# Attention scores in PSUM: two halves of 288 columns, or 512 and 64 side by side

## What is computed

```python
scores = scale * np.matmul(q, k.transpose(0, 1, 3, 2))
thresh = np.max(scores, axis=-1, keepdims=True) - tau
scores = np.where(scores >= thresh, scores, -1000000000.0)
attn = np.exp(scores - np.max(scores, axis=-1, keepdims=True))
attn = attn / (np.sum(attn, axis=-1, keepdims=True) + 1e-09)
x = np.matmul(attn, v)                  # heads side by side: 2304 x 512

h = x @ w_in                            # 512 -> 2048
x = (h * np.tanh(softplus(h))) @ w_out  # -> 512

g, val = x @ w_gate, x @ w_val          # 512 -> 1536
out = (silu(g) * val) @ w_out2          # -> 512
```

## Time and profile before

| | before |
|---|---|
| median of 3 runs | 1256.94 us (1254.13 to 1261.06) |
| the profiled execution | 1252.67 us |
| its span, first to last instruction | 1250.8 us |
| mean granted TensorE clock | 0.977 |
| TensorE matmul, busy | 1172.3 us, 94% |
| TensorE weight load, busy | 1139.1 us, 91% |
| DVE, ACT, POOL busy | 573.6, 476.1, 530.4 us |

### The profile page before, as it was taken

One profiled execution on the slowest core, in us unless ns is written; L12 is line 12 of the kernel. 1 busy time (PEld: TensorE's weight loads), 2 busy tenths in 40 slices (PEclk: granted clock), 3 DMA queues, 4 the chain that ended last, 5 costly groups with the idle time before them and its releaser, 6 DMA issues.

```text
span 1250.8 us, 21818 instructions
## 1 busy us (share of the span) xinstructions
PE 1172.3 (94%) x8608; PEld 1139.1 (91%) x8608; DVE 573.6 (46%) x1208; ACT 476.1 (38%) x873; POOL 530.4 (42%) x698
## 2 busy tenths in 40 slices
PE   1767689999999999999999998999999999999998
PEld 0656579999999999999999998999999999999998
DVE  3777741566677650355666653035666410002220
ACT  1555454334444244434454324433444304302210
POOL 4455568656677734323434523432443304301210
PEclk9777799999999999999999999999999999999999
DMA  7111147666656555444444454544433455444443
GB/s 240 44 30 44 49 125 250 220 200 204 193 198 186 204 170 168 154 132 144 148 137 141 136 161 137 175 151 143 137 116 120 135 195 178 169 164 162 166 166 106
DMA packets 83253, 190.69 MB, mean 152 GB/s; under 512 B 29392, under 2 KB 29392, under 8 KB 83152
## 3 DMA queue, kind: packets, MB, share of 16 engines
q1 hardware_dynamic: 83152, 189.30, 46.9%
HBM read 148.90 MB, written 40.37 MB: 151 GB/s over the span
## 4 chain that ended last, share of the span: by engine, by line
PE 88%; DVE 4%; ACT 2%; POOL 2%; issue 1%; DMA 1%; SPq 1%; DVEq 0%; ACTq 0%
PE ps_m L451 23%; PE ps_m L453 23%; PE ps_m L452 23%; PE ps_x L508 5%; PE ps_x L522 4%; PE ps_s L477 3%; PE ps_x L523 3%; PE ps_s L478 3%; DVE p_t L711 1%; DVE p_lo_b L723 1%; DMA k_raw<-kt 1%; PE ps_x L504 1%; DVE nmax L703 1%; ACT p_t L625 1%; DVE p_lo L723 1%
## 5 line engine op out<-in xcount | busy, mean ns | idle before, releaser
L451 PE MATMUL ps_m<-x_hi,w_sp 128*128 128x288 f32 x1280 | 379.9, 297 | 6.0 <-ACT g_raw L646 3.4
L453 PE MATMUL ps_m<-x_hi,w_sp 128*128 128x288 f32 x1280 | 378.0, 295 | 0.0
L452 PE MATMUL ps_m<-x_lo,w_sp 128*128 128x288 f32 x1280 | 377.3, 295 | 0.0
L451 PE MATMUL ps_m<-g_hi,w_sp 128*128 128x288 f32 x896 | 265.3, 296 | 0.0
L453 PE MATMUL ps_m<-g_hi,w_sp 128*128 128x288 f32 x896 | 264.2, 295 | 0.0
L452 PE MATMUL ps_m<-g_lo,w_sp 128*128 128x288 f32 x896 | 263.9, 295 | 0.0
L451 PEld LDWEIGHTS ps_m<-x_hi,w_sp 128*128 128x128 f32 x1280 | 240.5, 188 | 8.0 <-ACT g_raw L646 4.3
L453 PEld LDWEIGHTS ps_m<-x_hi,w_sp 128*128 128x128 f32 x1280 | 240.5, 188 | 0.0
L452 PEld LDWEIGHTS ps_m<-x_lo,w_sp 128*128 128x128 f32 x1280 | 240.5, 188 | 0.0
L451 PEld LDWEIGHTS ps_m<-g_hi,w_sp 128*128 128x128 f32 x896 | 168.2, 188 | 0.3
L452 PEld LDWEIGHTS ps_m<-g_lo,w_sp 128*128 128x128 f32 x896 | 168.1, 188 | 0.0
(11 more groups left out here) (79 smaller groups left out, 1548.3 us busy)
## 6 DMA issues: line engine op xcount, KB each, us to landing
w_sp<-scratch SPq DMA_DIRECT2D x204, 512.0 KB, 3.3
scratch<-w_sp SPq DMA_DIRECT2D x68, 512.0 KB, 2.9
w_raw<-weights SPq DMA_DIRECT2D x68, 256.0 KB, 3.4
q_raw<-qt SPq DMA_DIRECT2D x64, 144.0 KB, 3.7
k_raw<-kt SPq DMA_DIRECT2D x64, 144.0 KB, 3.7
out_t<-o_sb SPq DMA_DIRECT2D x16, 288.0 KB, 4.2
v_raw<-v SPq DMA_DIRECT2D x32, 128.0 KB, 2.4
v_raw<-v SPq DMA_DIRECT2D x32, 32.0 KB, 2.8
```

The costliest lines, as they stand in the source:

```text
L451: nc.tensor.matmul(ps, w_h, x_h, start=first, stop=False)
L452: nc.tensor.matmul(ps, w_h, x_l, start=False, stop=False)
L453: return nc.tensor.matmul(ps, w_l, x_h, start=False, stop=last)
```

## The change

The two score places are now seen as one run of 576 columns across two neighbouring banks: 512 columns fill the first bank and 64 lie at the start of the second. The matmuls of a chunk write columns 0 to 511 and 512 to 575 in place of 0 to 287 and 288 to 575 of each bank pair. Their number is the same, four for each head of a chunk, and so is the order of steps on every engine, since the planner's numbers are as before. `rowmax`, `exp` and `mask` take the 576 columns as one contiguous run.

```diff
-        def halves(ap):
-            return ap.rearrange("p (h t) -> p h t", h=2)
-
+        s_flat = ps_s.rearrange("p b t -> p (b t)")[:, 0:SEQ]
+        s_alone = ps_m.rearrange("p b t -> p (b t)")[:, BANK:BANK + SEQ]
...
         def s_banks(C):
             alone = C < CHUNKS * PAIRS
-            return ps_m[:, 1:3, 0:HALF] if alone and C % 2 else ps_s[:, :, 0:HALF]
+            return s_alone if alone and C % 2 else s_flat
...
-                for half in range(2):
-                    to = s_banks(C)[:, half, :]
-                    cols = slice(half * HALF, (half + 1) * HALF)
+                for cols in (slice(0, BANK), slice(BANK, SEQ)):
+                    to = s_banks(C)[:, cols]
                     for e in heads:
                         q = q_sp[:, e, q_columns(e, ci)]
                         nc.tensor.matmul(to, q, k_hi[:, e, cols], start=e == heads[0], stop=False)
...
-                act.activation(halves(p_t[:, slot, :]), s_banks(C), ACT.Exp, bias=nmax[:, slot:slot + 1]).then_inc(e_ready, 1)
+                act.activation(p_t[:, slot, :], s_banks(C), ACT.Exp, bias=nmax[:, slot:slot + 1]).then_inc(e_ready, 1)
...
-                dve.tensor_reduce(nmax[:, slot:slot + 1], s_banks(C), axis=AX.XY, op=ALU.max, negate=True).then_inc(max_ready, 1)
+                dve.tensor_reduce(nmax[:, slot:slot + 1], s_banks(C), axis=AX.X, op=ALU.max, negate=True).then_inc(max_ready, 1)
...
-                p = halves(p_t[:, slot, :])
+                p = p_t[:, slot, :]
```

## The result

The changed kernel takes 1277.28 us in the median of its first four runs, the kernel before 1256.51: a ratio of 1.0163 with a 95% interval of 1.013 to 1.0196. Slower, by 20.8 us. Five more runs of the same kernel gave 1276.91 us and 1.0158 (1.0135 to 1.0181). Every ratio in this document is against executions of the kernel before made beside the run in question, whose medians lay between 1256.4 and 1258.7 us.

What follows compares the result with a forecast made beforehand. PE was taken to bound the middle stage, a chain through all engines the first. 17.8 + 2.8 = 20.6 us on the 1256.94 us median gave 1277.5 us, range 1264 to 1291.

Steps and rivals of the forecast that it cites:

- head-chunk: 128 queries of one head against 576 keys, four score matmuls on PE; forecast 646 to 716 ns at full clock against 530.
- the short slot: PE's start-to-start time after a 64-column score matmul: 110 to 132 ns, because it must hold the next weights' load.
- 188 - 78 = 110 ns: Lower bound for a 64-column matmul's slot: score-weight load duration of 188 ns less 78 ns overlap, taken from the short transposes.
- Middle stage: Later batches' attention woven into the MLP matmuls, 168.2 to 980 us: 118 x 151 ns = 17.8 us longer (13.7 to 21.9).
- the 6.3 us that the prediction read: All the time PE waited while attention was woven into the MLP, none for the score chain; too little to hide the growth.
- First stage: Batch 0's attention alone, 26.8 to 168.2 us, bound by a chain through all engines: 2.8 us longer, bounds 0 to 14.9.
- three head-chunks of ten: Those the chain of waits passes in one pair of heads in batch 0's attention: 0.71 us a pair, times four.
- 0.28 for a half-clock chunk: Growth in us in batch 0's attention where another engine waits: 354 ns less 74 ns of last-matmul latency, 280 ns.
- Contiguous operands: Row maximum, exp and mask reading one run of 576 columns: no gain taken, at most 66 ns per exp, 2.4 us.
- The 60 ns slot: Rival: 64-column score matmuls nearly as cheap as short transposes, 1259 to 1262 us; chance 0.10 together with PE time swallowed by waits.
- columns alone: Rival: PE slots cost only their columns, nothing for the load; 480 ns per head-chunk, up to 9.1 us faster, 1248 us; chance 0.03.
- PE's time disappears in waits: Rival: idle PE time absorbs the longer score matmuls, so no change; chance 0.10 together with the 60 ns case.

Runs made afterwards that it cites:

- the additional matmuls: The kernel before with two unused 64-column matmuls more per head-chunk: 1286.11 us (1.0249) with weights of 128 columns, 1277.23 us (1.0171) with weights of 64.
- the cuts at 384 and 448: The changed kernel's contiguous place, cut as 384 + 192 and as 448 + 128 columns: 1262.06 us (1.0037) and 1268.58 us (1.0095) against the kernel before.
- the alternating order: The changed kernel with its matmuls ordered k_hi 512, k_hi 64, k_lo 512, k_lo 64, so no two short ones follow each other: 1277.50 us, ratio 1.0166.
- the kernel with the new scores in all the rest: 512 + 64 columns for all chunks but the 36 of batch 0, which keep two halves of 288: ratio 1.0125 against the kernel before, +15.7 us.
- Timed alone: 512 + 64 columns for the 36 chunks of batch 0 only, two halves of 288 elsewhere: ratio 1.0048 against the kernel before, +6.0 us.
- 320 + 256: The changed kernel's contiguous place, cut after 320 columns instead of 512: 1255.33 us, ratio 0.999 against the kernel before.
- 64 + 512: The changed kernel with the short matmuls first, columns 0 to 63 ending the first bank and 512 in the second: 1283.58 us, ratio 1.0219.

## Why the prediction was right, and where it was not

The forecast of 1277.5 us met 1277.28, with +20.6 forecast and +20.8 measured. The mechanism was right; that the two agree within 0.2 us is luck, since the difference is known to some 4 us either way (1.013 to 1.0196) and two deviations in a head-chunk cancel.

- **A head-chunk costs 646 to 716 ns, middle 681, +151.** Right: +148 ns in the distance above. The parts: 230 ns for 512 columns (forecast 213 to 226, a little under), 110 ns for 64 (forecast 110 to 132, at its lower end). The two deviations, +2 x 11 against the middle of one and -2 x 11 against that of the other, cancel. The 12 ns over the columns are not a fixed price: slots at full clock were 132 for 288 columns, 175 for 384 and 230 for 512, that is 12, 15 and 17 ns over 0.417 ns a column.
- **What holds the short slot is the load of the next weights.** Right, and shown by the additional matmuls (110 and 57 ns for loads of 128 and 64 columns behind the same 64 moving ones), the cuts at 384 and 448, and the alternating order. The conclusion from 188 - 78 = 110 ns hit the value itself. The sentence that no row shows the load's throughput holds for the rows chosen, not for the trace, as the pair of loads at 276.75 us shows.
- **Middle stage 17.8 us, nothing hides it.** 118 x 148 ns = 17.5 us by the measured growth; 15.7 (12.3 to 19.0) timed, 17.7 (16.2 to 19.2) at equal clock. In the traces it grew by 15.6, 19.3 and 19.7 us (the change twice, then the kernel with the new scores in all the rest), mostly as the half-clock stretches fell. In the first pair 1.3 us of the difference is the half-clock stretch after the pause, which the changed kernel's first execution missed, so 16.9; the other 0.6 us went into two pauses on PE, for g_raw and for p_lo, which were 3.4 and 0.5 us in the earlier trace rows and are now 3.0 and 0.2. The third pause there, for x_lo, ends at the first MLP matmul and so belongs to the first stage; 2.4 of the 6.3 us that the prediction read are, by this cut, not of the middle stage:

```profile
PE ps_m L451 <- ACT g_raw L645: 3.0, 1, 3.0
PE ps_m L451 <- POOL x_lo L839: 2.2, 1, 2.2
PE ps_x L507 <- DVE p_lo L722: 0.2, 1, 0.2
```

- **First stage 2.8 us.** Inside the bounds of 0 to 14.9; whether the value chosen was right stays open. Timed alone it is 6.0 us (3.6 to 8.3), at equal clock 4.1 (2.9 to 5.2); what the whole change leaves over the 17.5 us of the middle stage is 3.3 us as timed and 2.5 at equal clock. The weak step is the count, "three head-chunks of ten", read from one pair of one execution and not tested. The price of one was rather too high. Half clock, the kernel before and then the changed one, a chunk alone:

```profile
111.01 0.61 PE L477 MATMUL ps_m<-k_hi,q_sp 128*128 128x288 f32 x1 [0.26 <-DVE p_t L711]
...
111.89 0.44 PE L478 MATMUL ps_m<-k_lo,q_sp 128*128 128x288 f32 x1
```
```profile
42.13 0.79 PE L476 MATMUL ps_s<-k_hi,q_sp 128*128 128x512 f32 x1 [2.25 <-DVE p_t L710]
42.72 0.63 PE L477 MATMUL ps_s<-k_lo,q_sp 128*128 128x512 f32 x1
43.15 0.26 PE L476 MATMUL ps_s<-k_hi,q_sp 128*128 128x64 f32 x1
43.22 0.40 PE L477 MATMUL ps_s<-k_lo,q_sp 128*128 128x64 f32 x1
```

  From start to the end of the last: 1.32 us and 1.49, +0.16 to 0.17 (0.79 and 0.87, +0.08, at full clock), where I had 0.28 for a half-clock chunk that another engine waits for. The last short slot is mostly the load for the next matmul, and only who queues behind on PE pays for that. With 0.16 on three chunks of a pair one comes to 1.9 us, on all of the 36 to 5.8; the measured 2.5 to 6 lie between. How many are on the path was not shown chunk by chunk: the chain in the profile is one path of one execution, and when scores grow, branches that were almost as late take over. How much of the 6.0 us is this and how much the granted clock, whose half-clock stretches fall elsewhere in each execution, is settled only as far as the fit goes.
- **Contiguous operands: nothing.** Right to the nanosecond. The two reasons given, the price of 64 more columns and that of exp's bias, were not tested one by one.
- **The rivals.** The 60 ns slot and columns alone are refuted (110 ns measured). The Trainium skill, page "TensorE: Matmul & The Clock Gate", section "Back-to-back issue gap", gives N/2.4 + 2.5 ns for a matmul alone, which would have made the change free; this stream of load and matmul pairs does not follow it (230 ns measured for 512 columns, 110 for 64). The same page of the Trainium skill, section "LDWEIGHTS (loading the stationary operand)", gives P/1.2 ns for P columns of weights; the estimates from it, 107 ns for 128 columns and 53 for 64, are near the 110 and 57 measured. That PE's time disappears in waits is refuted as well: 17.5 us are added to its queue, and 17.7 (16.2 to 19.2) arrive.
- **The sum.** The middle stage came out at its term (17.5 for 17.8) and the first at or somewhat over its own (2.5 to 6 for 2.8). The bare times of the two halves, 15.7 and 6.0 us, suggest two errors that cancel, but the granted clock of those groups of executions explains most of that.

## What to carry to other kernels

When every matmul brings its own weights, cut the moving columns evenly: a slot lasts at least as long as the load of the weights that follow it. Here that is 110 ns for 128 fp32r columns at full clock, or, as an estimate from the slots measured, some 240 moving columns. The time by which a long matmul outlasts its load can't be lent to a short one. Filling a bank to 512 to leave a remainder of 64 costs 74 ns for each short matmul in this kernel (148 ns a head-chunk); 320 + 256 costs nothing. To price such a slot, measure from a matmul before the group to one well behind it, since the recorded starts of short matmuls lie before their weights are there. And before the times of two kernels that differ by a few us are set against each other, compare their mean granted clocks: 0.004 of it went with some 2 us here.

## What the runs showed of the hardware

- fp32r weight loads follow each other every 110 ns at full clock for 128 columns and every 50 to 60 ns for 64, though one is shown as 188 and 130 to 140 ns long. Only the next one runs ahead of a matmul (1480 ns for the alternating order, 1476 for the other). Columns do not settle it for every kind of load: those of the 64-column transposes have 128 columns too and follow each other every 60 ns; why is open.
- A matmul behind a short one is shown as started 30 or 110 ns after it and then as 0.09 us longer; its columns wait for the weights.
- Slots of 288, 384 and 512 columns at full clock are 132, 175 and 230 ns, at half clock exactly 240 for 288 columns. The surplus over 0.417 ns a column at full clock grows with the columns: 12, 15 and 17 ns.
- The granted clock fell after the same pause of 3.0 to 3.6 us in 12 of the 14 profiled executions: not in the first execution of the change and not in that of 64 + 512, whose pauses of 3.0 us others had as well. Two executions of one program differed by 5.1 us in the attention that runs alone.
